# A longer lead of constant products on TensorE, a pair of them ahead of each score level, and one load and one copy moved forward

## The chip, the cores and the metric

The kernel runs on one core of a Trainium2 chip. The metric is the device time of one execution in microseconds (us); the median of three runs stands for a kernel. Engines are named as in the profile: PE is TensorE's matmul part and PEld its weight load, DVE is VectorE, ACT is ScalarE, POOL is GpSimd, and SP is SyncE, which here only issues DMAs.

## The reference

Three stages follow each other, all in float32, for 4 batches of 768 tokens. In the first, each of 8 heads carries a 48x48 state through the tokens:

```python
for t in range(S):
    state = f[:, :, t, :, None] * state + np.einsum('bhd,bhe->bhde', k[:, :, t], v[:, :, t])
    y[:, :, t] = np.einsum('bhd,bhde->bhe', q[:, :, t], state)      # f = sigmoid(f_logit)
```

The second is a layer norm and a two-layer network with a residual: `x + relu(norm(x) * g_ln @ w_ch1) @ w_ch2`, 384 to 1536 to 384 channels. The third is `h = relu(x @ w_in)`, a convolution of 3 taps along the tokens, and `(h * sigmoid(conv)) @ w_out`, 384 to 1024 to 384 channels.

## The kernel before

**Units.** The tokens are cut into 8 units of 384, each of 3 chunks of 128. Stage one of a unit is a tree: the score of a query and a key needs the product of all gates between them, and the kernel builds these products by doubling. Level `st` (0 to 5) scores blocks of `2 << st` tokens. DVE multiplies half of the keys (`pK`) and of the queries (`pQ`) by the running gate products (`pT`), TensorE forms 96 small score products for a unit (`score`), and DVE (`mask`, levels 0 to 2) or ACT (`copy`, levels 3 to 5) takes them out of PSUM. So each level is a chain from DVE to TensorE and back. After the last level, `ktr` transposes a chunk's keys, `ktok` (ACT) copies them out, `kv` adds the chunk to the state, and `y` and `yend` form the chunk's output; `yend` raises the semaphore `y_done`. For unit 0, `xadd` is a copy on ACT of a chunk's output out of PSUM into X. `norm`, `xn`, `xnt`, `xh` and `xl` are the layer norm, its transpose and its split in a high and a low float32r part. `up`, `hhi`, `hlo` and `down` are the two-layer network in groups of 128 hidden channels.

**The start.** Unit 0 is worked in two parts: chunk 0 alone (written `.a` in the tables) and chunks 1 and 2 (`.0`). Its first scores have no gates in them: `even` and `odd` (the function `token`) score the even and the odd queries against the raw keys, and `self` moves part of them into place. Meanwhile the weights of stage two arrive in 12 pieces (`W0` to `W11`, 384 KB each) and are split: `whi` (ACT) rounds a piece to its high part, `wsub` (TensorE, two products of 128x128 by 384, one of them plain float32) forms piece minus high part in PSUM for half a piece, and `wlo` (ACT) copies it out. Pieces 8 and up are split by DVE (`wlv`).

**The order** of all this is written out by hand. `START` is a list of steps; a step is `name` + number + `.` + unit (`.a` and `.0` for the parts of unit 0). Each engine walks the same list and issues the steps of which it has a part, in that order, so a step that waits holds back all behind it on its engine. `LOADS` is the same for SP's queue: `K`, `Q`, `F`, `V` are a unit's keys, queries, gate inputs and values (`F0.2` is the gate input of unit 2), `N` a chunk of the inputs for the products of a token with its neighbour (`near`), `W` a weight piece. `gates` is ACT's sigmoid over F, in place; F has one buffer. The first of its two steps for unit 2, `gates0.2`, stands between `xadd1.0` and `xh0.0` on ACT.

**What makes a load wait.** F0.2 waits until DVE has used the gates of unit 1 (`prep_ready`, the step `pQ0.1`) and for `y_done` (line 450). `W7` waits for `wsub7`, `N1.1` for the third `y_done` of unit 0.

**Products of a constant tile.** The function `warm` is in TensorE's table of steps, but the list before does not name it. Its product is 128x128 by 384 in float32r, from HLO[:, 0], which DVE fills with 1.0 first of all, into the PSUM bank yb, whose first other use is `ktr0.0`; nothing reads the result.

After the start, the steady order (`PERIOD`) runs stages one and two of successive units beside each other, and then the third stage follows over 7 tiles of 440 tokens.

Of the kernel before, what the change touches and what calls it, by code (L numbers as in the profile page):

```python
# [129 lines left out]
def build(nc, q, k, f, v, near, g_ln, w1, w2, w3, cw, w4, x2d, out):  # L130
    with ExitStack() as ctx:
# [3 lines left out]
        def sem(name):  # L135
# [35 lines left out]
def phase_a(nc, sbuf, sem, bank, pair, q, k, f, v, near, g_ln, w1, w2, x2d, w3, cw, w4):  # L171
    with ExitStack() as own:
# [99 lines left out]
        y_done = sem("y_done")  # L272
# [38 lines left out]
            WJ.append((w2v[:, r, :], W2H[:, r, :], W2L[:, r, :]))  # L311
        NW, NW1 = len(WJ), len(WJ) - 6
        NPE = 8

        def half_of(ap, h):

            return ap[:, h % 2] if len(ap.shape) == 3 else ap[:, DM * (h % 2):DM * (h % 2) + DM]
# [41 lines left out]
        def placed(text):  # L359

            return [(steps(word.split(".")[0])[0], word.split(".")[1]) for word in text.split()]

        START = placed("""
            gates1.a gates1.0 even0.a whi0.0 diag0.0 even0.0 baseK0.a baseK0.0 baseQ0.a odd0.a baseQ0.0 pT0.a
            odd0.0 whi1.0 pT0.0 self0.a wsub0.0 wlo0.0 wsub1.0 wlo1.0 score0.a wlo2.0 gates0.1 score0.0 pQ0.0
            wsub2.0 pQ0.a self0.0 pK1.a wsub3.0 gates1.1 score1.0 whi2.0 wsub4.0 score1.a whi3.0 pK1.0
            score2.0 wlo3.0 copy3.0 pT1.a score2.a wsub5.0 whi4.0 score3.a pT1.0 mask0.0 score3.0 mask0.a
            pQ1.0 pQ1.a baseK0.1 copy3.a near0.1 pK2.0 pT2.0 wlo4.0 mask1.0 pQ2.0 pK2.a pT2.a score4.0 mask1.a
            score4.a pQ2.a pK3.0 pK3.a score5.0 mask2.a whi5.0 pT3.a pT3.0 score5.a pQ3.a wsub6.0 ktr0.0
            copy4.0 pQ3.0 wsub7.0 wlo5.0 mask2.0 pK4.a pK4.0 pT4.0 pT4.a pQ4.0 copy4.a wsub8.0 score0.1  # L370
            baseQ0.1 y0.0 pK5.0 pQ4.a pT5.0 copy5.0 wlo6.0 kv0.0 pQ5.0 yend0.0 pK5.a wlo7.0 pT5.a pQ5.a pK6.0
            ktok0.0 pK6.a pT6.0 pT6.a wlo8.0 neary0.1 copy5.a pQ6.a pQ6.0 wsub9.0 pT0.1 pQ0.1 nsum0.1 ktr1.0
            wsub10.0 score1.1 pK1.1 wlo9.0 xadd0.0 ktok1.0 mask0.1 y1.0 pT1.1 kv1.0 pQ1.1 yend1.0 wsub11.0
            st0.0 xnt0.0 norm0.0 y2.0 wlo10.0 pow0.0 xadd1.0 pK2.1 sscale1.0 xn0.0 st1.0 mask1.1 pT2.1
            sscale2.0 pQ2.1 xl0.0 gates0.2 yend2.0 xh0.0 score2.1 ktr2.0 whi6.0 wsub12.0 kv2.0 xadd2.0
            wsub13.0 norm1.0 wsub14.0 xnt1.0 score3.1 wsub15.0 norm2.0 mask2.1 ktok2.0 xacc0.0 xnt2.0 pow1.0
            xn1.0 pK3.1 st2.0 pT3.1 pQ3.1 pow2.0 near1.1 xacc1.0 xl1.0 xn2.0 score4.1 pK4.1 pT4.1 wlo11.0
            up0.0 up1.0 pQ4.1 nsum1.1 xacc2.0 whi7.0 wlv8.0 score5.1 wlo12.0 azero0.2 whi8.0 xl2.0 down0.0
            up2.0 pK5.1 up3.0 up4.0 neary1.1 baseK0.2 wlo13.0 ktr0.1 y0.1 pT5.1 xh1.0 gates1.2 copy3.1 pQ5.1
            hlo0.0 baseQ0.2 kv0.1 pK6.1 xh2.0 pT6.1 pow0.1 hlo1.0 wlv9.0 hlo2.0 yend0.1 pQ6.1 sscale0.1  # L380
            wlo14.0 pT0.2 wlv10.0 hlo3.0 pQ0.2 down1.0 score0.2 wlo15.0 wlv11.0 down2.0 xadd0.1 whi9.0 st0.1
            mask0.2 ktr1.1 pK1.2 copy4.1 hhi0.0 y1.1 kv1.1 sscale1.1 whi10.0 pT1.2 hhi1.0 pQ1.2 yend1.1
            copy5.1 up5.0 norm0.1 xadd1.1 pow1.1 score1.2 down3.0 whi11.0 down4.0 up6.0 hhi2.0 hhi3.0 st1.1
            ktok0.1 ktok1.1 xnt0.1 score2.2 near2.1 hlo4.0 hhi4.0 down5.0 neary2.1 pK2.2 mask1.2 xn0.1 pT2.2
            pQ2.2 up7.0 up8.0 ktr2.1 y2.1 hhi5.0 norm1.1 hlo5.0 hlo6.0 kv2.1 xh0.1 hhi6.0 pK3.2 yend2.1
            down6.0 hhi7.0 xl0.1 up9.0 down7.0 mask2.2 sscale2.1 hlo7.0 pow2.1 hhi8.0 ktok2.1 hhi9.0 nsum2.1
            down8.0 pT3.2 hlo8.0 score3.2 st2.1 xn1.1 xadd2.1 hlo9.0 down9.0 copy3.2 pQ3.2 pK4.2 pT4.2 norm2.1
            up10.0 hhi10.0 xnt1.1 score4.2 xh1.1 pQ4.2 hlo10.0 copy4.2 up11.0 down10.0 xl1.1 pK5.2 hhi11.0
            pT5.2 pQ5.2 xn2.1 hlo11.0 xl2.1 xh2.1 xnt2.1 xout0.0 down11.0 xout1.0 score5.2 xout2.0 pK6.2 pT6.2
            copy5.2 pQ6.2  # L390
            """)

        LOADS = placed("""
            G0.0 W0.0 K0.0 Q0.0 F0.0 Q0.1 W1.0 W2.0 K0.1 V0.0 V0.1 F0.1 W3.0 W4.0 W5.0 W6.0 N0.1 W7.0 F0.2 N1.1 W8.0 K0.2 W9.0 W10.0 W11.0 Q0.2 N2.1 V0.2 Q0.3 F0.3 N0.2 K0.3
            """)

        def part_of(where):
# [41 lines left out]
        def stage(j):  # L439
            a = STAGE[j % NS]  # L440
            return a.rearrange("p (a b) -> p a b", a=WJ[j][0].shape[1]) if len(WJ[j][0].shape) == 3 else a

        def sync(sp):
            def load_f(u, _):
                if not u.first:
                    sp.wait_ge(prep_ready[0], u.count(PREPS, 1 - PREPS))
                if u.index == 1:
                    sp.wait_ge(prep_ready[1], 1)
                if u.index == 2:
                    sp.wait_ge(y_done, 2)  # L450
                part = REST if u.first else WHOLE
                sp.dma_start(F[:, part], f[u.batch(), u.half, :, part]).then_inc(f_in, 16)

# [28 lines left out]
            def load_w(_, j):  # L482
                if j >= NS:

                    if j - NS < NPE:
                        sp.wait_ge(wp_done, 2 * (j - NS + 1))
                    else:
                        sp.wait_ge(wd_ready, j - NS - NPE + 1)
                sp.dma_start(stage(j), WJ[j][0]).then_inc(w_in[j % NS], 16)
# [56 lines left out]
        def gpsimd(pool):  # L546
# [61 lines left out]
            def neary(u, c):  # L608
# [131 lines left out]
        def vector(dve):  # L740
# [113 lines left out]
            def xadd(u, c):  # L854
# [4 lines left out]
                if c == 0:  # L859
                    dve.wait_ge(x_free, u.count(1, 1))  # L860
                    if u.index == 1:
                        dve.wait_ge(wp_done, 2 * NPE)
                        dve.wait_ge(wd_ready, NS - 1)
# [72 lines left out]
        def tensor(pe):  # L936
# [17 lines left out]
            def warm(_, i):  # L954

                if i == 0:
                    pe.wait_ge(still_ready, 1)
                for _ in range(2):
                    mm(yb[:, 0:T], HLO[:, 0, 0:P], HLO[:, 0], start=True, stop=True)

            def token(p, which):
# [160 lines left out]
            def up(u, g):  # L1122
# [4 lines left out]
                if u.first:  # L1127
                    pe.wait_ge(wl_ready, 2 * NPE)
                    if NW1 > NPE:
                        pe.wait_ge(wd_ready, NW1 - NPE)  # L1130
# [6 lines left out]
            def down(u, g):  # L1137
# [253 lines left out]
```

## Time and profile before

| | us |
|---|---|
| median of three runs (lowest, highest) | 725.72 (725.55, 727.74) |
| the profiled execution | 729.54 |
| its span | 727.5 |
| TensorE busy in the span | 696.6 (96%) |
| VectorE busy | 476.9 (66%) |
| ScalarE busy | 311.6 (43%) |
| mean granted TensorE clock | 0.979 of 2.4 GHz |

The span runs from the first to the last instruction of the profiled execution; the time has about 2 us more around it. "Busy" counts matmuls, loads of weights and element-wise instructions, not waits. The granted clock is 1.00 at 2.4 GHz and 0.50 at 1.2 GHz. The releaser of a wait is inferred from semaphores; "issue" is idle time for which the profile shows no releaser.

### The profile page before, as it was taken

To read this page: it belongs to the slowest core of one execution; us is meant where nothing else is said; L and a number is where in the kernel's file an instruction comes from. 1 tells how busy PE (TensorE), PEld (TensorE's weight loads), DVE (VectorE), ACT (ScalarE), POOL (GpSimd) and SP (SyncE) were. 2 spreads that over 40 slices of the span, in tenths; PEclk is the share of its full clock that TensorE was granted. 3 is DMA by queue.
4 is the path that set the end of the run, shared out by engine and by line. 5 is a ranking of instruction groups with operands and counts; after the bars stand their busy time and mean duration, and the time that the engine had idled before them with its cause. 6 is when DMAs were issued, how large, how long until landed. Compare 5 with 4: busy or idle time off the path is not lost.

```text
span 727.5 us, 21762 instructions
## 1 busy us (share of the span) xinstructions
PE 696.6 (96%) x9616; PEld 651.1 (90%) x9616; DVE 476.9 (66%) x885; ACT 311.6 (43%) x604; POOL 157.3 (22%) x178
## 2 busy tenths in 40 slices
PE   4878899999999999999999999999999999999998
PEld 3556699999999999999999999999989999999997
DVE  2774886557765856765865863435387777777764
ACT  3262631341242251261151142224477676776764
POOL 4021503143333423423414414500000000000000
PEclk9769999999999999999999999999999999999999
DMA  8322520432152133332342112135010120220111
GB/s 330 128 99 97 180 90 3 186 121 100 59 196 108 59 128 116 120 121 90 106 170 88 57 57 88 57 103 179 33 38 31 45 75 1 75 75 1 37 39 38
DMA packets 23231, 67.71 MB, mean 93 GB/s; under 512 B 3809, under 2 KB 14817, under 8 KB 23137
## 3 DMA queue, kind: packets, MB, share of 16 engines
q1 hardware_dynamic: 23136, 66.32, 26.5%
q8 instruction: 76, 1.25, 0.7%
q14 instruction: 19, 0.15, 0.1%
HBM read 56.86 MB, written 9.45 MB: 91 GB/s over the span
## 4 chain that ended last, share of the span: by engine, by line
PE 90%; DVE 5%; issue 2%; DMA 2%; ACT 1%; SPq 0%; DVEq 0%; ACTq 0%
PE bank L1118 14%; PE bank L1120 13%; PE bank L1119 13%; PE bank L1313 9%; PE bank L1015 9%; PE bank L1315 9%; PE bank L1314 9%; PE bank L1037 4%; DMA F<-f 2%; PE bank L1089 2%; PE bank L1059 2%; PE bank L1031 1%; PE bank L951 1%; PE bank L1112 1%; PE bank L1100 1%
## 5 line engine op out<-in xcount | busy, mean ns | idle before, releaser
L705 ACT ACTIVATE HHI<-bank 128x384 fp32r<-128x384 f32 x96 | 47.2, 492 | 160.0 <-PE bank L1120 159.7
L1290 DVE SCALAR_TENSOR_TENSOR TB<-HB,CW,TB 128x440 f32<-128x440 f32 x112 | 75.8, 677 | 50.2 <-ACT TB L1253 48.2
L917 DVE SCALAR_TENSOR_TENSOR HLO<-bank,HHI 128x384 fp32r<-128x384 f32 x96 | 53.2, 554 | 83.7 <-ACT HHI L705 83.7
L1118 PE MATMUL bank<-HHI,W2H 128*128 128x384 f32 x288 | 100.6, 349 | 0.0
L1118 PE MATMUL bank<-XH,W1H 128*128 128x384 f32 x288 | 99.1, 344 | 0.0
L1120 PE MATMUL bank<-XH,W1L 128*128 128x384 f32 x288 | 96.5, 335 | 0.0
L1120 PE MATMUL bank<-HHI,W2L 128*128 128x384 f32 x288 | 96.5, 335 | 0.0
L1119 PE MATMUL bank<-XL,W1H 128*128 128x384 f32 x288 | 96.4, 335 | 0.0
L1119 PE MATMUL bank<-HLO,W2H 128*128 128x384 f32 x288 | 96.4, 335 | 0.0
L793 DVE TENSOR_TENSOR K<-K,TOT 128x768 f32<-128x768 f32 (+2 forms) x54 | 56.7, 1052 | 47.4 <-PE bank L1015 37.0
L1015 PEld LDWEIGHTS bank<-Q,K 48*64 48x64 f32 x3840 | 65.9, 144 | 22.0 <-issue 21.9
L1015 PE MATMUL bank<-Q,K 48*64 48x32 f32 x3840 | 70.7, 228 | 10.6 <-DVE Q L804 7.0
L1313 PE MATMUL bank<-GHI,W4H 128*128 128x440 f32 x168 | 61.0, 363 | 0.6 <-DVE GLO L1303 0.6
L1313 PE MATMUL bank<-XBH,W3H 128*128 128x442 f32 x168 | 61.2, 364 | 0.3 <-ACT HB L1251 0.3
L1315 PE MATMUL bank<-XBH,W3L 128*128 128x442 f32 x168 | 61.0, 363 | 0.0
L1314 PE MATMUL bank<-XBL,W3H 128*128 128x442 f32 x168 | 60.9, 363 | 0.0
L1315 PE MATMUL bank<-GHI,W4L 128*128 128x440 f32 x168 | 60.7, 361 | 0.0
L1314 PE MATMUL bank<-GLO,W4H 128*128 128x440 f32 x168 | 60.6, 361 | 0.0
L1118 PEld LDWEIGHTS bank<-HHI,W2H 128*128 128x128 f32 x288 | 54.0, 188 | 1.6
L1118 PEld LDWEIGHTS bank<-XH,W1H 128*128 128x128 f32 x288 | 54.0, 188 | 1.1
L1119 PEld LDWEIGHTS bank<-HLO,W2H 128*128 128x128 f32 x288 | 54.1, 188 | 0.0
L1119 PEld LDWEIGHTS bank<-XL,W1H 128*128 128x128 f32 x288 | 54.1, 188 | 0.0
(127 smaller groups left out, 1373.5 us busy)
## 6 DMA issues: line engine op xcount, KB each, us to landing
NEAR<-near SPq DMA_DIRECT2D x21, 960.0 KB, 4.7
Q<-q SPq DMA_DIRECT2D x7, 768.0 KB, 4.3
K<-k SPq DMA_DIRECT2D x7, 768.0 KB, 4.9
F<-f SPq DMA_DIRECT2D x7, 768.0 KB, 6.1
V<-v SPq DMA_DIRECT2D x8, 576.0 KB, 6.9
x2d<-X SPq DMA_DIRECT2D x8, 576.0 KB, 4.4
XB<-x2d SPq DMA_DIRECT2D x6, 663.0 KB, 5.9
out<-OB SPq DMA_DIRECT2D x6, 660.0 KB, 4.4
```

The lines of the kernel that those rows point to most:

```text
L705: nc.scalar.activation(HHI[:, g % RA], ub[g % 2][:, 0:T], ACT.Relu).then_inc(hh_ready, 1)
L793: tt(blocks(Kc, 1 << st, 0), blocks(Kc, 1 << st, 0), spread(p, st, 1), ALU.mult)
L917: nc.vector.scalar_tensor_tensor(out=HLO[:, g % RA], in0=ub[g % 2][:, 0:T], scalar=0.0, in1=HHI[:, g % RA].bitcast(F32), op0=ALU.max, op1= ...
L1015: ins = mm(scores[half, par, at:at + QUARTER], K[u.par][rows, c, j, half], right[:, :, 1, :], start=True, stop=True)
L1037: return mm(pair[u.first][half, par, D * j:D * j + D], scores[keys, c, h], V[u.par][keys, c, D * h:D * h + D], start=start, stop=True, ski ...
L1118: mm(dst, ah, bh, start=start, stop=False, **kw)
L1119: mm(dst, ah, bl, start=False, stop=False, **kw)
L1120: return mm(dst, al, bh, start=False, stop=stop, **kw)
L1290: nc.vector.scalar_tensor_tensor(out=TB[:, g % RB], in0=HB[:, g % RB, tap:tap + TB_], scalar=CW[:, g, tap:tap + 1], in1=TB[:, g % RB], op0 ...
L1313: mm(dst, ah, bh, start=start, stop=False, **kw)
L1314: mm(dst, ah, bl, start=False, stop=False, **kw)
L1315: return mm(dst, al, bh, start=False, stop=stop, **kw)
```

## The change

- TensorE's list gets 20 steps `warm0` to `warm19`. `warm0` stands ahead of everything and has 20 products; each of the others has two. Two steps each (1 to 6) stand before `even0.0`, `odd0.a` and `odd0.0`, one (7) before `wsub0`, and one before each score step of unit 0 (8 to 19), of both parts.
- `F0.2` is moved ahead of `W7` in SP's queue, and waits for the first `y_done` (chunk 0's `yend0.0`) and no more for the second (`yend1.0`).
- `xadd0.0`, the copy of chunk 0's output on ACT, is moved from behind `wlo9.0` to ahead of it.

All other steps keep their order on every engine. The order of TensorE's first steps, and of ACT's around the copy, before and after:

```
TensorE before: even0.a even0.0 odd0.a odd0.0 wsub0 wsub1 score0.a score0.0 wsub2 wsub3 score1.0
                wsub4 score1.a score2.0 score2.a wsub5 score3.a score3.0 score4.0 score4.a score5.0 score5.a
                wsub6 ktr0.0 wsub7 wsub8 score0.1 y0.0 kv0.0 yend0.0 wsub9 ktr1.0 wsub10 score1.1 ...
TensorE after:  warm0 even0.a warm1 warm2 even0.0 warm3 warm4 odd0.a warm5 warm6 odd0.0 warm7 wsub0 wsub1
                warm8 score0.a warm9 score0.0 wsub2 wsub3 warm10 score1.0 wsub4 warm11 score1.a warm12 score2.0
                warm13 score2.a wsub5 warm14 score3.a warm15 score3.0 warm16 score4.0 warm17 score4.a
                warm18 score5.0 warm19 score5.a wsub6 ktr0.0 ... (as before)
ACT before:     ... wlo8 copy5.a wlo9 xadd0.0 ktok1.0 wlo10 xadd1.0 gates0.2 xh0.0 whi6 xadd2.0 ktok2.0 near1.1 wlo11 whi7 ...
ACT after:      ... wlo8 copy5.a xadd0.0 wlo9 ktok1.0 (as before)
```

```diff
         NPE = 8
+        WARM_FIRST = 20
...
-            G0.0 W0.0 K0.0 Q0.0 F0.0 Q0.1 W1.0 W2.0 K0.1 V0.0 V0.1 F0.1 W3.0 W4.0 W5.0 W6.0 N0.1 W7.0 F0.2 N1.1 W8.0 K0.2 W9.0 W10.0 W11.0 Q0.2 N2.1 V0.2 Q0.3 F0.3 N0.2 K0.3
+            G0.0 W0.0 K0.0 Q0.0 F0.0 Q0.1 W1.0 W2.0 K0.1 V0.0 V0.1 F0.1 W3.0 W4.0 W5.0 W6.0 N0.1 F0.2 W7.0
+            N1.1 W8.0 K0.2 W9.0 W10.0 W11.0 Q0.2 N2.1 V0.2 Q0.3 F0.3 N0.2 K0.3
...
                 if u.index == 2:
-                    sp.wait_ge(y_done, 2)
+                    sp.wait_ge(y_done, 1)
...
                 if i == 0:
                     pe.wait_ge(still_ready, 1)
-                for _ in range(2):
+                for _ in range(WARM_FIRST if i == 0 else 2):
                     mm(yb[:, 0:T], HLO[:, 0, 0:P], HLO[:, 0], start=True, stop=True)
```

## Rows read from the trace of the kernel before

**Rows 1.** The page: busy time, share of the span and instructions of each engine.

```profile
PE 696.6 (96%) x9616; PEld 651.1 (90%) x9616; DVE 476.9 (66%) x885; ACT 311.6 (43%) x604; POOL 157.3 (22%) x178
```

**Rows 2.** Busy time by stretch: length, five engines (instructions), granted clock, DMA share, GB/s.

```profile
0.00:19.33 19.33, 9.29 (x198) 7.31 (x198) 5.80 (x12) 6.28 (x11) 8.12 (x27) 1.00 0.87 324
19.33:26.16 6.83, 3.99 (x127) 3.07 (x127) 5.87 (x16) 2.85 (x5) 0.00 (x0) 1.00 0.74 258
26.16:50.05 23.89, 18.89 (x435) 15.34 (x428) 18.25 (x45) 10.72 (x25) 3.46 (x3) 0.50 0.20 71
...
56.88:60.29 3.41, 3.41 (x43) 2.52 (x38) 0.89 (x2) 0.03 (x1) 0.00 (x0) 0.50 0.02 5
60.29:80.77 20.48, 15.49 (x466) 11.72 (x467) 13.47 (x33) 9.49 (x18) 6.61 (x7) 1.00 0.54 185
80.77:84.19 3.42, 3.42 (x63) 2.65 (x56) 1.97 (x4) 1.88 (x4) 0.00 (x0) 0.50 0.02 5
...
100.00:727.50 627.50, 621.81 (x7901) 590.00 (x7895) 409.83 (x748) 268.90 (x519) 132.81 (x136) 1.00 0.25 84
```

**Rows 3.** Timeline of TensorE, the first 30 us: start, duration, instruction, idle before.

```profile
5.90 1.08 PE L972 MATMUL bank<-Q,K 48*64 48x32 f32 x32 [5.90 <-DMA Q<-q]
10.68 2.78 PE L972 MATMUL bank<-Q,K 48*64 48x32 f32 x96 [3.70 <-DMA Q<-q]
13.81 1.93 PE L972 MATMUL bank<-Q,K 48*64 48x32 f32 x64 [0.34 <-DVE K L756]
```

**Rows 4.** The chain that ended last, 0 to 130 us: start, duration, what.

```profile
11.88 1.06 ACT F L653
...
30.23 3.60 PE bank L1015 x128
...
35.73 2.92 PE bank L1015 x96
...
49.37 0.32 PE bank L952
...
51.84 0.17 PE bank L952
52.01 1.53 PE bank L1015 x96
...
53.69 2.32 issue
...
65.84 5.31 DMA F<-f
```

**Rows 5.** Timeline of ACT, 0 to 100 us.

```profile
38.67 1.49 ACT L676 COPY ATD<-bank 16x256 f32<-16x256 f32 x4 [10.87 <-PE bank L1015]
...
71.18 0.63 ACT L653 ACTIVATE F<-F 128x512 f32<-128x512 f32 x1 [4.91 <-DMA F<-f]
...
73.73 0.52 ACT L658 ACTIVATE NEAR<-NEAR 128x384 f32<-128x384 f32 x1
```

**Rows 6.** Timeline of DVE, 0 to 100 us.

```profile
61.16 0.56 DVE L890 BATCH_NORM_STATS2 BN<-X 128x6 f32<-128x384 f32 x1 [3.39 <-ACT X L687]
...
72.21 0.56 DVE L913 TENSOR_TENSOR XL<-bank,XH 128x384 fp32r<-128x384 f32 x1 [4.79 <-ACT XH L700]
```

**Rows 7.** Timeline of TensorE, 60 to 100 us.

```profile
75.88 0.88 PE L951 MATMUL bank<-YN,ID 128*128 128x384 f32 x2
...
78.42 0.52 PE L1100 MATMUL bank<-ID,XN 128*128 128x128 f32 x3 [1.48 <-DVE ST L886]
80.00 2.18 PE L1015 MATMUL bank<-Q,K 48*64 48x32 f32 x96 [1.06 <-DVE Q L804]
```

**Rows 8.** Waits of SP, 0 to 100 us: total, times, longest.

```profile
SPq L450 <- PE bank L1037: 14.2, 1, 14.2
```

**Rows 9.** The load of N1.1, issued at 69.02 us: KB, us to landing.

```profile
NEAR<-near SPq DMA_DIRECT2D x1, 960.0 KB, 4.7
```

**Rows 10.** DMA queues between 53.6 and 54.7 us: packets, MB, share.

```profile
q8 instruction: 1, 0.02, 5.4%
```

More of the change, by code:

```diff
@@ L363, in phase_a @@
         START = placed("""
[L364 to L388, printed above, removed]
@@ L389, in phase_a @@
-            pT5.2 pQ5.2 xn2.1 hlo11.0 xl2.1 xh2.1 xnt2.1 xout0.0 down11.0 xout1.0 score5.2 xout2.0 pK6.2 pT6.2
-            copy5.2 pQ6.2
+            warm0.0 gates1.a gates1.0 even0.a warm1.0 warm2.0 whi0.0 diag0.0 even0.0 warm3.0 warm4.0 baseK0.a
+            baseK0.0 baseQ0.a odd0.a warm5.0 warm6.0 baseQ0.0 pT0.a odd0.0 warm7.0 whi1.0 pT0.0 self0.a
+            wsub0.0 wlo0.0 wsub1.0 wlo1.0 warm8.0 score0.a wlo2.0 gates0.1 warm9.0 score0.0 pQ0.0 wsub2.0
+            pQ0.a self0.0 pK1.a wsub3.0 gates1.1 warm10.0 score1.0 whi2.0 wsub4.0 warm11.0 score1.a whi3.0
@@ new lines, in phase_a @@
+            pK1.0 warm12.0 score2.0 wlo3.0 copy3.0 pT1.a warm13.0 score2.a wsub5.0 whi4.0 warm14.0 score3.a
+            pT1.0 mask0.0 warm15.0 score3.0 mask0.a pQ1.0 pQ1.a baseK0.1 copy3.a near0.1 pK2.0 pT2.0 wlo4.0
+            mask1.0 pQ2.0 pK2.a pT2.a warm16.0 score4.0 mask1.a warm17.0 score4.a pQ2.a pK3.0 pK3.a warm18.0
+            score5.0 mask2.a whi5.0 pT3.a pT3.0 warm19.0 score5.a pQ3.a wsub6.0 ktr0.0 copy4.0 pQ3.0 wsub7.0
+            wlo5.0 mask2.0 pK4.a pK4.0 pT4.0 pT4.a pQ4.0 copy4.a wsub8.0 score0.1 baseQ0.1 y0.0 pK5.0 pQ4.a
@@ new lines, in phase_a @@
+            pT5.0 copy5.0 wlo6.0 kv0.0 pQ5.0 yend0.0 pK5.a wlo7.0 pT5.a pQ5.a pK6.0 ktok0.0 pK6.a pT6.0 pT6.a
+            wlo8.0 neary0.1 copy5.a xadd0.0 pQ6.a pQ6.0 wsub9.0 pT0.1 pQ0.1 nsum0.1 ktr1.0 wsub10.0 score1.1
+            pK1.1 wlo9.0 ktok1.0 mask0.1 y1.0 pT1.1 kv1.0 pQ1.1 yend1.0 wsub11.0 st0.0 xnt0.0 norm0.0 y2.0
+            wlo10.0 pow0.0 xadd1.0 pK2.1 sscale1.0 xn0.0 st1.0 mask1.1 pT2.1 sscale2.0 pQ2.1 xl0.0 gates0.2
+            yend2.0 xh0.0 score2.1 ktr2.0 whi6.0 wsub12.0 kv2.0 xadd2.0 wsub13.0 norm1.0 wsub14.0 xnt1.0
@@ new lines, in phase_a @@
+            score3.1 wsub15.0 norm2.0 mask2.1 ktok2.0 xacc0.0 xnt2.0 pow1.0 xn1.0 pK3.1 st2.0 pT3.1 pQ3.1
+            pow2.0 near1.1 xacc1.0 xl1.0 xn2.0 score4.1 pK4.1 pT4.1 wlo11.0 up0.0 up1.0 pQ4.1 nsum1.1 xacc2.0
+            whi7.0 wlv8.0 score5.1 wlo12.0 azero0.2 whi8.0 xl2.0 down0.0 up2.0 pK5.1 up3.0 up4.0 neary1.1
+            baseK0.2 wlo13.0 ktr0.1 y0.1 pT5.1 xh1.0 gates1.2 copy3.1 pQ5.1 hlo0.0 baseQ0.2 kv0.1 pK6.1 xh2.0
+            pT6.1 pow0.1 hlo1.0 wlv9.0 hlo2.0 yend0.1 pQ6.1 sscale0.1 wlo14.0 pT0.2 wlv10.0 hlo3.0 pQ0.2
@@ new lines, in phase_a @@
+            down1.0 score0.2 wlo15.0 wlv11.0 down2.0 xadd0.1 whi9.0 st0.1 mask0.2 ktr1.1 pK1.2 copy4.1 hhi0.0
+            y1.1 kv1.1 sscale1.1 whi10.0 pT1.2 hhi1.0 pQ1.2 yend1.1 copy5.1 up5.0 norm0.1 xadd1.1 pow1.1
+            score1.2 down3.0 whi11.0 down4.0 up6.0 hhi2.0 hhi3.0 st1.1 ktok0.1 ktok1.1 xnt0.1 score2.2 near2.1
+            hlo4.0 hhi4.0 down5.0 neary2.1 pK2.2 mask1.2 xn0.1 pT2.2 pQ2.2 up7.0 up8.0 ktr2.1 y2.1 hhi5.0
+            norm1.1 hlo5.0 hlo6.0 kv2.1 xh0.1 hhi6.0 pK3.2 yend2.1 down6.0 hhi7.0 xl0.1 up9.0 down7.0 mask2.2
@@ L391, in phase_a @@
+            sscale2.1 hlo7.0 pow2.1 hhi8.0 ktok2.1 hhi9.0 nsum2.1 down8.0 pT3.2 hlo8.0 score3.2 st2.1 xn1.1
+            xadd2.1 hlo9.0 down9.0 copy3.2 pQ3.2 pK4.2 pT4.2 norm2.1 up10.0 hhi10.0 xnt1.1 score4.2 xh1.1
+            pQ4.2 hlo10.0 copy4.2 up11.0 down10.0 xl1.1 pK5.2 hhi11.0 pT5.2 pQ5.2 xn2.1 hlo11.0 xl2.1 xh2.1
+            xnt2.1 xout0.0 down11.0 xout1.0 score5.2 xout2.0 pK6.2 pT6.2 copy5.2 pQ6.2
             """)
         LOADS = placed("""
-            G0.0 W0.0 K0.0 Q0.0 F0.0 Q0.1 W1.0 W2.0 K0.1 V0.0 V0.1 F0.1 W3.0 W4.0 W5.0 W6.0 N0.1 W7.0 F0.2 N1.1 W8.0 K0.2 W9.0 W10.0 W11.0 Q0.2 N2.1 V0.2 Q0.3 F0.3 N0.2 K0.3
+            G0.0 W0.0 K0.0 Q0.0 F0.0 Q0.1 W1.0 W2.0 K0.1 V0.0 V0.1 F0.1 W3.0 W4.0 W5.0 W6.0 N0.1 F0.2 W7.0
```

## The prediction, made before the changed kernel was run

> **What bounds the kernel now.** I read the page first, then busy time by stretch, the chain that ended last, and the timelines of single engines around what the change touches. TensorE is busy for 96% of the span [rows 1], and from 100 us to the end it is idle for only 627.50 - 621.81 = 5.7 us [rows 2]. So from 100 us on the kernel is TensorE's own work, at the high clock, and a microsecond saved ahead of it moves the end by a microsecond. What is left to win lies in the first 100 us, in two forms. The first is idle time: TensorE idles for 727.5 - 696.6 = 30.9 us in all [rows 1], so some 25 us of that lie in the first 80 us (from 80 to 100 it never idles). The second is a clock at its lower level: 26.16 to 50.05, 56.88 to 60.29 and 80.77 to 84.19 us are granted 0.50 [rows 2]. The row for 0 to 19.33 says 1.00, but the durations contradict it: 32 products of 48x32 take 1.08 us there [rows 3], 34 ns each, and the same kind takes 2.92 / 96 = 30 ns in a stretch at 0.50 and 1.53 / 96 = 16 ns at 1.00 [rows 4]. I read the start as low until 19.33 us, too.
>
> What the engine did before the clock moved: it fell at 26.16 after 6.83 us with 3.99 us of work [rows 2], and at 56.88 after the idle 2.32 us at 53.69 [rows 4]. It rose at 60.29 after a stretch of 3.41 us without any idle time. Score products, 128 of them from 30.23 and 96 from 35.73 with only one weight step between [rows 4], did not lift it although TensorE was never idle there; full 128x128 products were part of what ran ahead of each rise.
>
> **Price of the products.** A float32r product of 128x128 by 384 takes 0.32 us at the low and 0.17 us at the high clock [rows 4]. The list adds 20 and 19 x 2 = 58 of them: 18.6 us at the low, 9.9 us at the high clock, if nothing hid them.
>
> **The first 20.** They start when DVE has filled HLO, near 1.4 us, and last at most 20 x 0.32 = 6.4 us, until 7.8. The first tokens start at 5.90 now [rows 3] and would slip by up to 1.9 us, but what follows them waits for the second Q load until 10.68 [rows 3], and the next gates are ready only from 11.88 + 1.06 = 12.94 [rows 4]. Cost 0; without that cover 1.9. Steps 1 and 2 (four products, 0.7 to 1.3 us) fit in the same wait.
>
> **Tokens and the first half-levels.** Now `even0.0`, `odd0.a` and `odd0.0` run from 10.68 to 13.81 + 1.93 = 15.74 [rows 3], and DVE's `baseQ0.0` waits for their end; from there DVE's chain leads to each level. At the high clock the 160 products take 2.6 us and the eight of steps 3 to 6 take 1.4; the last third cannot start before DVE's keys are ready at 13.7, so it ends near 14.8: a gain of 0.9 us, and 0.1 to 0.2 more in score0.0. Taken: 1.0. At the low clock the eight products cost 8 x 0.32 = 2.6 less the present gap of 0.34: a loss of 2.3. These are the two ends.
>
> **Levels 1 to 5, 26 to 50 us.** TensorE works 18.89 us there at 0.50 [rows 2]; at 1.00 this is 9.4. It can't all be won, because the levels alternate with DVE, and DVE has 18.25 us of work in the 23.89 [rows 2]. DVE's idle 5.6 us is the upper bound. What the levels wait for next is ACT: its run of copies that begins at 38.67 when score3.0 ends [rows 5] goes on without a gap for 6.5 us. Following the steps through with high-clock durations and a pair ahead of each score step (most pairs start while TensorE would wait for DVE, so only steps 11, 13 and 15 stand in its way, about 0.3 us each), score3.0 ends 4.5 us earlier and `y0.0` 5.5 us earlier, the second figure with the 1.0 from above. But there is a wait of some 2.6 us between score4.0 and score4.a in that schedule (now 2.4), longer than the idle that stood before the fall at 26.16. I expect the clock to fall there, or once more at 23 to 26 us, and take 3.0 of the 4.5. The lower end is a loss: if the clock stays low, steps 11 to 15, in the part where TensorE never idles now, cost 5 x 0.64 = 3.2 us.
>
> One page of the Trainium skill bears on this: TensorE: Matmul & The Clock Gate, section Part 1, says that the whole ramp penalty is below 1% of a typical kernel's span. By it, as an estimate, 7.3 us would be the most that all the clock's part could bring. No row shows that share; my sum below takes less than that for the clock.
>
> **56 to 60 us.** `yend0.0` and `wsub9` run in the 3.41 us at 0.50 [rows 2]; at 1.00 they take half, a gain of 1.7. That needs TensorE not to stand still for 2.32 us before it [rows 4]. Nothing releases that wait in the profile, and in the same moment one packet of the instruction queue moves [rows 10], just after the load of W7 which was issued at 51.22. I read it as an instruction fetch behind W7's load. The change puts W7 behind F0.2, thus later, so this stall may go (a gain of 2.3), but the two loads, 1152 KB, now start at `yend0.0`, and a fetch may fall into them (a loss of 2.3). I take 0 for the stall, both ends for the range, and 0.8 of the 1.7, half.
>
> The Trainium skill, Runtime: NRT & Kernel Launch, section Instruction fetch mechanics, says that crossing from one instruction page to the next is mostly hidden. By that the stall is something else and stays where it is; the row of the instruction queue speaks against it. It would leave my sum as it is.
>
> **F0.2.** It now waits 14.2 us for the second `y_done` [rows 8], is issued at 65.84 and takes 5.31 [rows 4]. ACT stands at `gates0.2` for 4.91 of them [rows 5], behind it `xh0.0`, behind that DVE with `xl0.0`, idle 4.79 [rows 6]. With the change it is issued at `yend0.0`, at 58.3 on the present clock, and lands near 63.6, before ACT comes to it at 66.3: the whole wait goes. What is late next is N1.1. It is issued at 69.02, after the third `y_done`, and takes 4.7 [rows 9], so ACT's near1.1 stays where it is, at 73.73 [rows 5], and behind it on ACT wlo11, whi7 and wlo12, for which wsub13 and wsub14 wait. So wsub14 stays at 75.88 [rows 7]; after it come only its 0.9 us, and xnt1 with 0.5. The present waits of 1.48 and 1.06 for DVE [rows 7] go, because DVE is 4 us ahead by then, so score3.1 starts near 77.4 and not at 80.00: 2.6. TensorE then idles 2.5 us less ahead of 80.77, and I expect no fall there: of the 3.42 us at 0.50 [rows 2] half is won, 1.7. Together 4.3; bounds 0.5 (N1.1 lands later, in the shadow of W7) and 5.
>
> **W7** has lots of room: its rounding runs at 74.5, and it would be issued at 58.7. **xadd0.0** lets DVE's norm0.0 start 2.3 us earlier than 61.16 [rows 6], but DVE's next step waits for score1.1, which ends at 63.1, either way: 0.
>
> **The sum.** 1.0 + 3.0 + 0.8 + 0 + 4.3 = 9.1 us off the profiled span of 727.5, so 718.4, and a time of 720.4 against 729.54. This execution is 3.8 us above the median of the runs shown, so in some of them a part of these losses was probably not there; I take 1.0 us off the gain. 725.7 - 8.1 = 717.6 us.
>
> **Rivals.**
> 1. The clock still falls early and stays low for most of 26 to 50 us, as it does now. For it: scores without idle time did not raise it, and TensorE waits 1.7 us ahead of score1.0 in the new schedule, against 1.9 now. Against it: the pairs are full products. Then the pairs of the continuous part cost about 2, the start and F0.2 still bring 1.0 + 4.3: 725.7 - 3.3 = 722.4. Chance 0.22.
> 2. The wait for F0.2 is replaced by that for N1.1 altogether, and the clock falls at 80 as before. It gives 0.5 in place of 4.3: 717.6 + 3.8 = 721.4. Chance 0.10.
> 3. More than forecast: no fall before 60 us, and the stall at 53.69 gone. 1.0 + 4.5 + 1.7 + 2.3 + 4.3 = 13.8, so 712 to 713. Chance 0.12.
> 4. Slower: the clock falls in the wait for the second Q load, where TensorE would have little to do from about 9 to 10.68, and the pairs run at the low clock from there. Cost 2.3 in the tokens, 3.2 in the levels, and 2.3 for a fetch behind the two loads, 7.8 in all, against the 4.3 of F0.2: 725.7 + 3.5 = 729.2. It decides when more than half of the 38 later products, each 0.32, stand in TensorE's way: 19 x 0.32 = 6.1, more than the 4.3 and the 1.0 together. Chance 0.08.
> 5. The parts cancel, or the clock is set by something else than the work ahead of it, and the load's gain is lost to a fetch: within 0.3% (2.2 us, about what a measurement of this kernel can tell from no change). Chance 0.05.
>
> **How the numbers follow.** The forecast itself, from 714 to 721, has 0.43. Faster by over 0.3% holds the forecast and rivals 1, 2 and 3, 0.87; within it 0.05; slower 0.08. The range leaves out rivals 4 and 5 and a part of 3 and of the upper end of 1: 712.5 to 723.5.
>
> **What the profile after would show.** Products of the new line from 1.4 us, and those after the first 4 to 7 us at 0.17 us apart; the three token steps ended near 14.8; no or a much shorter stretch at 0.50 between 26 and 50; F's load issued when `yend0.0` ends, without a wait of ACT at `gates0.2`; ACT waiting for NEAR instead, by up to 2 us; no stretch at 0.50 at score3.1. Wrong would be: score products at 30 ns with pairs at 0.32 between them; a long "issue" wait of TensorE while F0.2 and W7 are in flight; or a saving ahead of 80 us that is gone by 120 us because DVE or ACT falls behind TensorE there.

## The result and the profile after

The changed kernel is slower: a median of 736.4 us (731.5 to 739.2, 9 runs) against 727.8 us (725.2 to 731.5, 9 runs) for the kernel before, a ratio of 1.0127 with a 95% interval of 1.0099 to 1.0154. The forecast was 717.6. The profiled execution has a span of 732.1 us.

The page of the kernel after, part 1, beside [rows 1]:

```profile
PE 709.5 (97%) x9674; PEld 661.2 (90%) x9674; DVE 476.2 (65%) x885; ACT 311.9 (43%) x604; POOL 156.3 (21%) x178
```

TensorE has 58 products and 12.9 us of busy time more, and is idle for 22.6 us instead of 30.9. The other engines do what they did. Busy time by stretch, beside [rows 2]; columns as there:

```profile
0.00:5.11 5.11, 3.72 (x12) 3.72 (x13) 0.60 (x2) 1.92 (x2) 3.69 (x14) 1.00 0.55 176
5.11:11.93 6.82, 5.27 (x118) 4.39 (x120) 0.43 (x1) 0.81 (x1) 4.17 (x14) 1.00 0.99 387
11.93:22.17 10.24, 10.24 (x143) 7.96 (x143) 6.35 (x11) 3.94 (x9) 0.00 (x0) 0.50 0.76 286
...
29.00:32.41 3.41, 3.41 (x39) 2.37 (x37) 2.17 (x6) 0.40 (x2) 0.00 (x0) 0.50 0.02 5
32.41:42.65 10.24, 8.83 (x279) 6.68 (x275) 8.27 (x25) 3.15 (x8) 0.17 (x1) 1.00 0.39 138
42.65:52.89 10.24, 8.52 (x95) 6.17 (x94) 8.92 (x17) 6.00 (x15) 3.91 (x3) 0.50 0.01 2
...
63.13:69.96 6.83, 5.61 (x75) 4.30 (x74) 2.70 (x7) 1.01 (x2) 0.00 (x0) 0.50 0.01 2
...
114.33:117.75 3.42, 3.42 (x13) 3.38 (x13) 3.27 (x7) 0.00 (x0) 0.00 (x0) 0.50 0.02 5
100.00:732.10 632.10, 623.85 (x7912) 592.08 (x7906) 411.23 (x748) 269.07 (x519) 132.09 (x136) 1.00 0.24 83
```

The clock does rise early, at 5.11 us, as the first 20 products were to make it, and the long stretch at 0.50 from 26 to 50 us is broken up. But it falls at 11.93, after a stretch that holds a wait of 1.5 us for the second Q load (until 9.88), and there are falls where the kernel before had none. From 100 us on TensorE idles 632.10 - 623.85 = 8.3 us, not 5.7 [rows 2]. The chain that ended last shows where, beside [rows 4]: start, duration, what.

```profile
61.08 0.46 PE bank L1062 x27
61.54 2.81 issue
...
71.96 4.87 DMA NEAR<-near
76.85 0.52 ACT NEAR L661
...
107.35 0.49 PE bank L1092 x16
107.85 1.16 issue
...
111.45 1.52 PE bank L1018 x94
112.97 1.17 issue
```

TensorE stands still in the middle of `y1.0` for 2.81 us, and at about 108 and 113 us for 1.16 and 1.17, each time with no releaser. The wait of 2.32 us at 53.69 [rows 4] is gone: `y0.0` now follows score0.1 at once. All this is the same kind of wait, in other places. The first product of `up0.0`, behind all the added ones, starts at 86.44 us, and at 86.67 in the kernel before: the 4.6 us between the two profiled spans (732.1 and 727.5) are lost behind that point. The waits of TensorE over the whole span of the kernel after: total, times, longest.

```profile
PE bank L1062 <- issue: 2.8, 1, 2.8
PE bank L954 <- ACT W1L L728: 2.3, 1, 2.3
...
PE bank L1018 <- issue: 1.2, 1, 1.2
PE bank L1040 <- issue: 1.2, 1, 1.2
```

The load of F0.2 did what was forecast: it is issued when `yend0.0` ends, and ACT has no wait at `gates0.2`. The wait for N1.1 took the place of the wait for F0.2: issued at 71.96 it took 4.87 us, ACT waited 2.0 us for it, and TensorE 2.3 us for ACT behind it.

### The profile page after: what moved, and what is told of

The parts are those of the page before. It is cut to its first block, busy times and chain, and to the rows that moved or that the text cites. A ratio compares the mean times of both kernels' runs of the same rounds, so it can differ in the third digit from the quotient of the medians.

```text
span 732.1 us, 21878 instructions
## 1 busy us (share of the span) xinstructions
PE 709.5 (97%) x9674; PEld 661.2 (90%) x9674; DVE 476.2 (65%) x885; ACT 311.9 (43%) x604; POOL 156.3 (21%) x178
## 4 chain that ended last, share of the span: by engine, by line
PE 91%; DVE 4%; issue 2%; DMA 2%; ACT 1%; SPq 0%; DVEq 0%; ACTq 0%
PE bank L1121 14%; PE bank L1123 13%; PE bank L1122 13%; PE bank L1316 9%; PE bank L1318 9%; PE bank L1317 9%; PE bank L1018 8%; PE bank L1040 4%; PE bank L1062 2%; PE bank L954 2%; PE bank L1092 2%; PE bank L1034 1%; PE bank L962 1%; PE bank L1103 1%; PE bank L1011 1%
## 5 line engine op out<-in xcount | busy, mean ns | idle before, releaser
L1018 PEld LDWEIGHTS bank<-Q,K 48*64 48x64 f32 x3840 | 62.1, 137 | 19.0 <-issue 18.9
L1018 PE MATMUL bank<-Q,K 48*64 48x32 f32 x3840 | 67.0, 222 | 7.9 <-DVE Q L807 5.5
L1122 PEld LDWEIGHTS bank<-HLO,W2H 128*128 128x128 f32 x288 | 54.7, 190 | 0.0
L1123 PEld LDWEIGHTS bank<-XH,W1L 128*128 128x128 f32 x288 | 54.1, 188 | 0.7 <-issue 0.7
```

The costliest lines, as they stand in the source:

```text
L1018: ins = mm(scores[half, par, at:at + QUARTER], K[u.par][rows, c, j, half], right[:, :, 1, :], start=True, stop=True)
L1122: mm(dst, ah, bl, start=False, stop=False, **kw)
L1123: return mm(dst, al, bh, start=False, stop=stop, **kw)
```

## The experiments

All times are medians of 6 to 12 runs in one batch beside runs of the kernel before on the same chip, whose medians lay at 726.1 to 726.6 in the batches of e1 to e18. "Added" counts TensorE instructions more than in the kernel before; a product is two, a weight load and a matmul.

| | what | added | us | ratio to before (95%) |
|---|---|---|---|---|
| | the changed kernel | 116 | 736.4 | 1.0127 (1.0099 to 1.0154) |
| e1 | F0.2's load alone | 0 | 726.5 | 1.0011 (0.9987 to 1.0034) |
| e2 | changed, load back | 116 | 732.3 | 1.0102 (1.0059 to 1.0146) |
| e3 | first 20 alone | 40 | 727.9 | 1.0028 (1.0004 to 1.0051) |
| e4 | 116 increments | 116 | 738.6 | 1.0164 (1.0131 to 1.0198) |
| e5 | changed, 70 tiny | 256 | 731.2 | 1.0076 (1.0046 to 1.0105) |
| e6 | changed, all 58 tiny | 116 | 738.6 | 1.0160 (1.0119 to 1.0202) |
| e7 | changed, pairs only | 76 | 735.9 | 1.0114 (1.0071 to 1.0157) |
| e8 | changed, half tiny | 116 | 741.7 | 1.0207 (1.0171 to 1.0243) |
| e9 | before, 58 tiny first | 116 | 735.4 | 1.0119 (1.0090 to 1.0147) |
| e10 | before, 128 tiny first | 256 | 730.5 | 1.0067 (1.0043 to 1.0091) |
| e11 | F0.2 and near1.1 | 0 | 726.8 | 0.9996 (0.9977 to 1.0015) |
| e12 | before, 98 tiny first | 196 | 726.4 | 1.0002 (0.9985 to 1.0019) |
| e13 | changed, 60 tiny, pairs | 196 | 728.9 | 1.0019 (0.9989 to 1.0049) |
| e14 | e11, 98 tinier first | 196 | 723.2 | 0.9944 (0.9916 to 0.9972) |
| e15 | changed, 70 tinier first | 256 | 726.8 | 0.9988 (0.9958 to 1.0017) |
| e16 | before, 98 tinier first | 196 | 723.3 | 0.9950 (0.9926 to 0.9974) |
| e17 | before, 58 tinier first | 116 | 733.0 | 1.0102 (1.0058 to 1.0147) |
| e18 | before, 128 tinier first | 256 | 726.9 | 1.0007 (0.9986 to 1.0027) |

**Two theories.** A: the added instructions move the points at which TensorE's instruction stream is fetched, and a fetch that falls in a burst of small products stops the engine. C: the products' own time costs, where they stand in TensorE's way. B is a variant of A in which the moved load holds the fetch.

**e1, the load alone.**

```diff
-... N0.1 W7.0 F0.2 N1.1 ...        sp.wait_ge(y_done, 2)
+... N0.1 F0.2 W7.0 N1.1 ...        sp.wait_ge(y_done, 1)
```

> Only the load of F0.2 is changed (ahead of W7, first y_done); no added products. Theory A (what made the changed kernel slow is the added instructions on TensorE, which move the places where its instruction stream is fetched): this kernel keeps the gain forecast for F0.2, 2.5 to 4.3 us faster than before, without a wait of ACT at gates0.2. Theory B (F0.2 and W7, in flight together, hold back an instruction fetch): an issue wait of 2 us or more near 60 to 64 us and a time 0 to 4 us above before.

No gain and no loss: neither the gain that A expected nor the wait near 60 to 64 us that B did. Waits of TensorE in e1's profile:

```profile
PE bank L1037 <- issue: 2.4, 2, 1.7
PE bank L951 <- ACT W1L L725: 2.3, 1, 2.3
```

The first row holds the wait at `y0.0`, 1.7 us where it was 2.3. W7's load is issued only at 56.98 here, behind that wait: so between these two executions W7's load was at most 0.6 us of it, and theory B in my prediction's form (W7 holds the fetch) has little to carry. The second is the wait behind N1.1.

**e2, the changed kernel with the load back.**

```diff
-... N0.1 F0.2 W7.0 N1.1 ...        sp.wait_ge(y_done, 1)
+... N0.1 W7.0 F0.2 N1.1 ...        sp.wait_ge(y_done, 2)
```

> The changed kernel with the load of F0.2 put back; all 58 products and the copy stay. Theory A: still slower than before, by the changed kernel's 9 us plus the load's lost gain, 8 to 12 us. Theory B: the issue wait of 2.81 us at 61.5 us and the low clock after it are gone, and the time is that of before or up to 4 us faster.

Still 1.0% slower, 6.1 us: B is wrong, and A's 8 to 12 us was too much. The loss is in the products' part. The wait in `y1.0` stayed, 1.5 us long where it was 2.81; if the two loads lengthened it, one execution against another is all that shows it.

**e3, the first 20 alone.**

```diff
+            warm0.0 gates1.a ...
-                for _ in range(2):
+                for _ in range(20):
```

> The kernel before with the first 20 constant products alone (40 more instructions, all in the wait for the first loads). If products hidden in a wait cost nothing: within 1 us of before, or up to 1 us faster by the high clock at even0.0. Theory A: 40 more instructions move the fetches too, so 1 to 4 us slower or faster is possible, with issue waits at other places than 53.69 us. A rival C (the products themselves are the cost, where they stand in TensorE's way at the low clock): no loss here, since these 20 stand in nobody's way.

Slower by 0.28%, with an interval that just leaves out 1, though the products stand in nobody's way. The 40 instructions come with them, and this run can't tell the two apart.

**e4, the same number of instructions without matrix work.**

```diff
+            for _ in range(116):
+                pe.sem_inc(pad_sem, 1)
```

> The kernel before with 116 increments of an unused semaphore ahead of TensorE's list: as many instructions as the 58 products have (58 products and 58 weight loads), but no matrix work. Theory A: issue waits move to where the changed kernel has them (near score1.1 and y1.0, and near 108 and 113 us), and the time is 3 to 6 us above before. Theory C: the time is that of before within 1 us, as the increments lie in the first 5.9 us, where TensorE waits.

A flawed measurement: an increment took 0.16 us, so the first token product started at 19.0 us and not at 5.9, and the time says nothing clean. What it does show is the places: issue waits of 1.5 us in `y1.0` and of about 1.0 and 0.9 further on, and none at `y0.0`.

**e5 to e8: the changed kernel with other products in the same list.** In e5, 70 tiny products follow the first pair; in e6 every product is tiny; in e8 every second one. e7 drops the first 20.

```diff
+                for _ in range(70 if i == 1 else 0):                                  (e5)
+                    mm(yb[0:HALF, 0:16], HLO[0:HALF, 0, 0:HALF], HLO[0:HALF, 0, 0:16], start=True, stop=True)
-                    mm(yb[:, 0:T], HLO[:, 0, 0:P], HLO[:, 0], start=True, stop=True)  (e6)
+                    mm(yb[0:HALF, 0:16], HLO[0:HALF, 0, 0:HALF], HLO[0:HALF, 0, 0:16], start=True, stop=True)
-        WARM_FIRST = 20                                                               (e7)
+        WARM_FIRST = 0
-                for _ in range(WARM_FIRST if i == 0 else 2):                          (e8)
+                for _ in range(WARM_FIRST // 2 if i == 0 else 1):
+                    mm(yb[0:HALF, 0:16], HLO[0:HALF, 0, 0:HALF], HLO[0:HALF, 0, 0:16], start=True, stop=True)
```

> The changed kernel with 70 tiny products (64x64 by 16) more behind the first pair, in the wait for the second Q load: 58 + 70 products are 256 instructions more than in the kernel before, where the changed kernel has 116 more. Theory A (the places of the instruction fetches make it slow; they look one page of 256 instructions apart): the fetches lie as in the kernel before again, the issue waits at 108 and 113 us go, and the time falls by 4 to 8 us against the changed kernel, to 728 to 732. Theory C (the products' own time on TensorE): the time stays at 736 or rises by the tiny products' 2 us.

> The changed kernel, load and copy moved as well, with each of its 58 products cut from 128x128 by 384 to 64x64 by 16: as many instructions in the same places, almost no matrix work. Theory A: the issue waits at the changed kernel's places, and a time of 732 to 737. Theory C: the time of the kernel with the load moved alone, 726 to 728.

> The changed kernel without its first 20 products; the 19 pairs stay. Theory C: the 20 alone cost 2 us, the pairs the rest, so 733 to 735. Theory A: 76 more instructions than before put the fetches elsewhere than 116 do; the time can be anything from 727 to 736, and follows the issue waits. A third, D (a first long stretch at the high clock lifts nothing, because it ends in the wait for the second Q load): the low clock's time per execution is lower than with the 20.

> The changed kernel with every second of its products cut to 64x64 by 16: as many instructions in the same places, half the matrix work. Theory C: half of the products' cost is left, so a time midway between that of e6 and that of the changed kernel, near 731. Theory A: no different from the changed kernel, 734 to 737.

e6 has next to no matrix work and is as slow as the changed kernel or slower; e8, with half of it, is the slowest. C can't be the main cause. e5 has 70 products more than the changed kernel and starts its last token step 4.7 us later, and is 5.2 us faster. That speaks for A, with a period of 256 instructions. But A does not account for all of it. e6 came out above A's range (738.6 against 732 to 737): its score products take 32 ns each over its first 57 us, so it lost there by the low clock too. e8, at 741.7, missed A's 734 to 737 by more: its last token step starts at 18.39, 4.0 us later than in the changed kernel; the rest is open. e7 (one of its six runs took 743.5 us) shows that 76 instructions cost as much as 116, which A allows and doesn't foresee.

**e9, e10, e12: nothing but instructions ahead of the kernel before.** 58, 128 and 98 tiny products.

```diff
+            warm0.0 gates1.a ...
-                for _ in range(2):
-                    mm(yb[:, 0:T], HLO[:, 0, 0:P], HLO[:, 0], start=True, stop=True)
+                for _ in range(58):                                             (128, 98)
+                    mm(yb[0:HALF, 0:16], HLO[0:HALF, 0, 0:HALF], HLO[0:HALF, 0, 0:16], start=True, stop=True)
```

> The kernel before, its loads and copy unmoved, with 58 tiny products (64x64 by 16) ahead of TensorE's list: the 116 instructions of the change, all in the wait for the first loads, and next to no matrix work. Theory A (the fetches' places): 3 to 6 us above before, with issue waits of 1 to 1.5 us at y1.0 and at about 108 and 113 us and none at y0.0. Theory C (the products' own time and the clock): the time of before within 1 us.

> The kernel before with 128 such tiny products ahead of TensorE's list: 256 instructions, one whole page by theory A, so the fetches lie as in the kernel before and the time is that of before within 1 us, with the issue wait at y0.0 again. If instructions ahead of the list cost by their number, it is slower than the kernel with 116 instructions more.

> The kernel before with 98 tiny products ahead of TensorE's list, 196 instructions, 60 short of a page. Theory A: the fetches lie 60 instructions later than in the kernel before; issue waits move with them, and the time differs from before by some us in either direction: 723 to 731. Theory C: the time of before within 1 us.

e9 costs 1.19%, nearly all of what the whole change costs, 9.3 us where A expected 3 to 6. e10 was expected at the time of before and missed it by 4.4 us; its 128 products last until 15.2 us, so `odd0.0` starts at 18.93 where it started at 13.81 [rows 3], 5.1 us late. e18 below has the same 256 instructions without the late start and is at the time of before, so the start accounts for it. e12 starts the same step 1.9 us late and is not slower than before; both theories allowed that.

**e11, the load with near1.1 out of its way.**

```diff
-            xn1.0 pK3.1 st2.0 pT3.1 pQ3.1 pow2.0 near1.1 xacc1.0 ... whi7.0 wlv8.0 score5.1 wlo12.0 azero0.2
+            xn1.0 pK3.1 st2.0 pT3.1 pQ3.1 pow2.0 xacc1.0 ... whi7.0 wlv8.0 score5.1 wlo12.0 near1.1 azero0.2
```

> The kernel before with the load of F0.2 moved, and near1.1 moved from ahead of wlo11 to behind wlo12 in the list, so that ACT does not stand at the wait for N1.1 while wsub13 and wsub14 need wlo11 and wlo12. If the wait for N1.1 took the place of that for F0.2: TensorE's wait of 2.35 us for ACT is gone and it is 1 to 3 us faster than the load's move alone, thus 723 to 725. If the load was hidden anyway: no change, 726.

A miss, 726.8 against 723 to 725: of TensorE's wait of 2.3 us for wlo11 nothing is left in the profile, a wait of 1.2 us for a later `wlo` copy and one of 0.9 for `xn` stand in its place, and the time is that of before.

**e13 to e18: shorter tiny products (32x32 by 4), so that the start is not late.** e13 is the changed kernel with 60 of them in place of the first 20, e15 with 70 ahead of the 20; e16, e17 and e18 are the kernel before with 98, 58 and 128 ahead of the list; e14 is e11 with 98.

```diff
+                for _ in range(70 if i == 0 else 0):                                  (e15)
+                    mm(yb[0:QUARTER, 0:4], HLO[0:QUARTER, 0, 0:QUARTER], HLO[0:QUARTER, 0, 0:4], start=True, stop=True)
                 for _ in range(WARM_FIRST if i == 0 else 2):
```

> The changed kernel (load and copy moved, 19 pairs in their places) with 60 tiny products (32x32 by 4) in place of the first 20: 196 instructions more than the kernel before, the shift that brought no loss. Theory A alone (only the fetches' places cost): within 2 us of before, 725 to 728. Theory C besides A (the pairs cost their own time where they stand in TensorE's way): 728 to 732, which is the pairs' price by itself.

> The kernel before with the load of F0.2 moved, near1.1 behind wlo12, and 98 tiny products of 32x32 by 4 ahead of TensorE's list: 196 instructions. If a good shift and the load together bring what the load alone did not: 722 to 725. If the load is worth nothing wherever the fetches lie: the time of the kernel with 196 instructions alone.

> The changed kernel, whole, with 70 tiny products of 32x32 by 4 ahead of its first 20: 256 instructions more than before, one page. Theory A: the changed kernel's time less its fetch losses, 727 to 730, of which some 1 to 2 us are the later start of the first tokens. Theory C: 734 or more.

> The kernel before, nothing moved, with 98 products of 32x32 by 4 ahead of TensorE's list, 196 instructions. The same shift with 98 larger tiny products gave 726.4 with the first tokens 1.9 us late; if these are shorter, so that the start is not late, theory A expects 724.5 to 726; the time of before if the start never mattered.

> The kernel before with 58 products of 32x32 by 4 ahead of TensorE's list, 116 instructions, all done before the first tokens. The same product and place as in the kernel with 98 of them (723.3 us), only fewer. Theory A: slow, 730 to 736, with issue waits at y1.0 and at about 108 and 113 us. If the number of instructions does not matter: 723 to 727.

> The same with 128 products, 256 instructions, done near 8.5 us, before the second Q load. Theory A with a page of 256: the time of the kernel before within 1 us, 725.5 to 727.5. If a page were not 256, the time would be some other value of the range seen, 723 to 736.

e16, e17 and e18 differ in one number only: 196 added instructions gain 0.50%, 116 lose 1.02%, 256 do nothing. e15 does everything the change did, plus 70 products that do nothing, and the loss of 1.27% is gone (one of its 12 runs took 2349 us, which the median does not see). e15 alone would not settle it, because the 70 products also push the first 20 back: these end at 10.9 us, TensorE has no wait for Q, and its tokens ran at 18 to 21 ns each. In the two profiles this is worth little: `y0.0` starts at 53.7 in e15 and at 55.5 in the changed kernel, 1.8 us, while the spans differ by 10.4. The chain of e17, to be held against that of the changed kernel above:

```profile
105.44 0.49 PE bank L1089 x16
105.93 1.09 issue
107.02 0.68 PE bank L1037 x22
...
109.49 1.52 PE bank L1015 x94
111.01 1.15 issue
112.16 0.30 PE bank L1015 x2
```

TensorE stops behind the same 16 products of `kv`, and later behind the 94th of 96 score products, as the changed kernel does (its line for `kv` is L1092). What was added to the two kernels shares little but the count of instructions. Between the end of the first of these waits and the start of the second, e17 and the changed kernel do this; columns as in [rows 2], first e17, then the changed kernel:

```profile
105.95:111.05 5.10, 3.99 (x127) 3.62 (x127) 1.93 (x7) 0.76 (x2) 0.55 (x1) 1.00 0.06 20
```

```profile
107.90:113.00 5.10, 3.97 (x127) 3.56 (x127) 1.90 (x7) 0.73 (x2) 0.55 (x1) 1.00 0.04 13
```

That is 127 products and 127 weight loads, 254 instructions, in both, and instructions that only wait or signal are not in the row: the two waits lie about one page of 256 apart. The instruction queue fits, too. Over the whole span it moves 76 packets in the kernel before, the changed kernel, e16 and e17, and 77 in e15 and e18, the ones with 256 instructions more; TensorE's 2 x 9616 instructions [rows 1] are just over 75 times 256. First the kernel before, then e18:

```profile
q8 instruction: 76, 1.25, 0.7%
```

```profile
q8 instruction: 77, 1.26, 0.7%
```

In the stretch around each wait of e17 this queue moves one packet. DMA queues of e17 from 104.5 to 107 us and from 109.4 to 112:

```profile
q1 hardware_dynamic: 156, 0.62, 61.2%
q8 instruction: 1, 0.02, 2.5%
```

```profile
q8 instruction: 1, 0.02, 2.6%
```

In both stretches the packet moves ahead of the wait (by 105.5 and by 110.0 us), and how it leads to the wait is not shown. A packet alone makes no wait, either: e18 and e15 move three each between 100 and 112 us, and neither has a wait without a releaser there. TensorE's waits in e15, over the span:

```profile
PE bank L1020 <- DVE Q L807: 5.5, 7, 2.3
PE bank L954 <- ACT W1L L728: 2.8, 1, 2.8
...
PE bank L1042 <- issue: 1.3, 1, 1.3
```

Of the three long issue waits of the changed kernel, 5.1 us together, one is left, 1.3 us long.

As to what was expected: e14 came out at e16's time, as it would if the load is worth nothing; e15, e17 and e18 came out as A had it (e15 by 0.2 us below its range); e16 was 1.2 us better than that. e13 lies in the range in which the pairs have a price of their own besides A.

## Why the prediction was wrong

**The step that failed** is the price of the products. It counted their matrix time, 18.6 or 9.9 us, and looked for cover for it. It did not ask what 116 more instructions do to everything behind them. I had the right clue: the wait of 2.32 us at 53.69 with one packet of the instruction queue [rows 4, 10]. But I asked of it only whether W7's load was to blame, took 0 for it, and put its bounds at 2.3 either way, for one place. The runs show in its place: the same 116 instructions, hidden and nearly without work, cost 1.02% (e17), and 1.19% with a somewhat later start (e9), and moving the fetches on by a whole page gives the changed kernel the time of before (e15, 0.9988). 1.0127 less 0.9988 is 1.4%, 10 us. The two profiled spans differ by 10.4. Of that, the issue waits are 2.81 + 1.16 + 1.17 less the 1.31 that e15 keeps, 3.8, and the stretches at 0.50 that follow them, from 63.13 with 5.61 us of work and from 114.33 with 3.42, cost about half of it, 4.5: 8.3 us. (The stretches at 0.50 ahead of 60 us, three in the changed kernel and two in e15, are left out.) That the falls follow from the waits is argued from their order, not shown, and e17 has its waits at 106 and 111 us without a fall behind them.

With this step a premise fell: that a microsecond saved ahead of 100 us moves the end by one, because behind it all is TensorE's own work. From the first product of `up0.0` to the end it is 640.8 us in the kernel before, 645.7 in the changed kernel and 643.6 in e17, but 640.6 in e15 and 640.4 in e18.

The Trainium skill, Runtime: NRT & Kernel Launch, section Instruction fetch mechanics, has a refill block of 256 instructions. e17 and e18 agree with the 256. Its "mostly hidden" holds by the count of packets, 76 in a span with a few waits, but it was no ground for taking the cost as nothing: 96 score products are 192 instructions in 1.53 us [rows 4], and a fetch that falls there is not hidden.

**The first 20.** Their cost in the wait was forecast at 0, and e3 has 0.28% for them and the 40 instructions. The clock did rise, then fell before it was of much use: the high stretch from 5.11 to 11.93 holds the wait for Q; `even0.0` ran in it at 18 ns a product, and `odd0.a` and `odd0.0` behind it at 32 to 33. My gain of 1.0 for the front was the other end, a loss: score1.0 started at 27.62 in place of 25.8. (The loss end itself was added up slightly wrong: 2.56 less 0.34 is 2.2, not 2.3.) That was rival 4's mechanism at its place.

**Levels 1 to 5 and 56 to 60 us.** 3.0 and 0.8 us were forecast for the higher clock. This term was mis-sized, as e15 against e18 shows, both with 256 added instructions: all 58 products and the moved load together come to 726.8 against 726.9. In the profiles, one execution each, the clock did what the products were for: in e15's score products take 18 to 21 ns until 23 us, and in e18's they take 29 to 34 until 46 us. That the products' own time used up what this gave is argued, not shown. It can't be settled by the mean granted clock of the timed runs, because the granted clock does not see the start. In e18's profile it reads 1.00 up to 50.5 us, while 128 score products take 3.67 us, 29 ns each:

```profile
0.00:50.50 50.50, 42.01 (x873) 34.70 (x874) 30.21 (x71) 19.90 (x39) 11.24 (x30) 1.00 0.53 193
```

```profile
30.49 3.67 PE L1015 MATMUL bank<-Q,K 48*64 48x32 f32 x128
```

So what a microsecond at the low clock costs here stays open. One reason to expect less than half of it is in the prediction: from 26 to 50 us DVE has 18.25 us of work in 23.89 [rows 2].

**F0.2.** Forecast a gain of 4.3, measured a loss of 0.8 us (e1; from 0.9 faster to 2.5 slower by its interval) and, at a better shift, nothing again: e14 against e16 is 723.2 against 723.3. Held against the one profile that I had read, the mechanism came out, and even the size: in e1 N1.1 is issued at 67.98, TensorE waits 2.3 us behind it, score3.1 starts at 76.35 (forecast 77.4, before 80.00), and `up0.0` at 82.48 where it started at 86.67, 4.2 us earlier. (In the changed kernel N1.1 came later, at 71.96, behind the wait in `y1.0` and a stretch at 0.50, and score3.1 started at 80.31.) But the medians do not have this gain. The profiled execution of the kernel before took 729.54 us, 3.4 more than the median of e1's batch, and that of e1 724.4, 2.1 less than its own: I took 1.0 us off the whole sum for that, where nearly all of this term was due. The falls at 56.88 and 80.77 are not in every execution: by the mean granted clock, the lowest of 112 timed executions has about 3 us at 0.50, and each of the two is 3.4. With the wait behind N1.1 out of the way (e11) nothing came either; shorter ones took its place. In e14's profile `up0.0` starts at 78.40 and in e16's at 80.46, and e14 loses the 2.1 us again behind it: its clock is at 0.50 from 77 to 84 us. Whether that is so in most executions stays open.

**xadd0.0 and W7** were forecast at 0; nothing in the profiles contradicts it.

**Also open:** e13, pairs with 196 instructions added, is 5.6 us slower than e16. Its pairs ran at the low clock, 0.32 us each, up to 22 us and at the high clock behind that until 40. And the number of added instructions is the same as in e16 only behind the last pair: within the levels its fetches fall elsewhere. In its profile TensorE stands still for 3.78 us in `score4.0`, with 39 of its products ahead of the wait and 25 behind; apart from the start of e4 that is the longest wait without a releaser in any profile here:

```profile
44.88 0.87 PE L1020 MATMUL bank<-Q,K 48*64 48x32 f32 x25 [3.78 <-issue]
```

How the 5.6 us divide between that and the pairs' own time was not tried.

**A version that beats both** is e16: the kernel before with 98 products of 32x32 by 4 ahead of TensorE's list, 723.3 us, 0.5% faster than before. Against e17 and e18 only the number of products differs, so its gain hangs on where the fetches fall, and it must be found anew after any edit of TensorE's list. By which waits it gains is not shown: its profile has 4.0 us of them without a releaser, where that of the kernel before has 4.3.

## What to carry to other kernels

When an edit adds or removes instructions on an engine that runs bursts of very small ones, test it once more with a filler that brings the difference in instructions to 256, ahead of everything: what changes between the two is the place of the fetches and not the edit. An idle time with no releaser, about a page of instructions from another such, is the sign to look for; a packet of the instruction queue alone is none. And read how much of a term is there in every execution before adding terms from one: the moved load gained 4.2 us from one profile to another, and nothing from one median to another.

## What the runs showed of the hardware

- A wait that is read here as a fetch costs TensorE 1.09 to 1.17 us of standing still where it falls badly in the steady part (e17 and the changed kernel), 1.74 with the first loads in flight (e17, below), 2.81 with F0.2 and W7 in flight (the changed kernel), and 3.78 in e13's levels. From one such wait to the next, e17 and the changed kernel issue 254 products and weight loads.
- 196, 116 and 256 instructions ahead of the same list gave 723.3, 733.0 and 726.9 us (e16, e17, e18): a range of 9.7 us, 1.3%, with the same useful work.
- The granted clock of a profile can read 1.00 from the start although products take the time of the low level: up to 50.5 us in e18, and up to 57 us in e6.
- Very small products are not free: 58 of 32x32 by 4 took 3.25 us, 56 ns each (e17), and 58 of 64x64 by 16 6.35 us, 109 ns (e9), both at the start of the execution. A semaphore increment on TensorE's queue took 0.16 us: 116 of them fill the 19.05 us up to e4's first product.

The start of TensorE's timeline in e17:

```profile
1.39 3.25 PE L959 MATMUL bank<-HLO 32*32 32x4 f32 x58 [1.39 <-DVE HLO L741]
...
12.44 1.25 PE L972 MATMUL bank<-Q,K 48*64 48x32 f32 x34 [0.35 <-DVE K L756]
15.43 1.07 PE L972 MATMUL bank<-Q,K 48*64 48x32 f32 x30 [1.74 <-issue]
```
